# Expert stage of a fused scan, router and two feed-forward kernel: the order of routing work, written-out TensorE rounds, and split turns of the half tiles

## The reference

```python
for t in range(S):                      # 4 batches, 8 heads, 768 tokens, head size 48
    cur = einsum('bhd,bhe->bhde', u[None] * kt, vt)
    y[:, :, t] = einsum('bhd,bhde->bhe', rt, state + cur)
    state = wt[:, :, :, None] * state + einsum('bhd,bhe->bhde', kt, vt)
...
noisy = x @ w_gate + log1p(exp(x @ w_noise)) * noise   # x: 3072 x 384, 8 experts
top2, top2_w = the two best experts of each token, softmax over the two
for e in range(8):
    out[mask] += top2_w * (maximum(x[mask] @ w1[e], 0) @ w2[e])   # 384 -> 1024 -> 384
...
h = x @ w_in                            # 384 -> 2048
return (h - tanh(h)) @ w_out            # 2048 -> 384
```

## Time and profile before

| | us |
|---|---|
| median of 3 runs | 1153.69 (1153.0 to 1162.76) |
| the profiled execution, its own time | 1157.02 |
| its span | 1155.4 |
| TensorE busy | 1076.8 (93% of the span), 8738 matmuls |
| VectorE, ScalarE, GpSimd busy | 702.6, 542.3, 199.2 |

### The profile page before, as it was taken

One profiled execution on the slowest core, in us unless ns is written; L12 is line 12 of the kernel. 1 busy time (PEld: TensorE's weight loads), 2 busy tenths in 40 slices (PEclk: granted clock), 3 DMA queues, 4 the chain that ended last, 5 costly groups with the idle time before them and its releaser, 6 DMA issues.

```text
span 1155.4 us, 24252 instructions
## 1 busy us (share of the span) xinstructions
PE 1076.8 (93%) x8738; PEld 1029.8 (89%) x8738; DVE 702.6 (61%) x892; ACT 542.3 (47%) x754; POOL 199.2 (17%) x325
## 2 busy tenths in 40 slices
PE   4887968998999999999999999899999999999998
PEld 3776866997999999999999999799999999999997
DVE  8978876489677777776776777543434344333433
ACT  4344424564466666666666666333332332323232
POOL 2108675017800000000000000401010110101010
PEclk9989889999899999999999999999999999999999
DMA  7645535859888888888888888301010110101010
GB/s 128 157 101 125 138 102 179 271 161 328 271 282 281 272 286 272 283 274 271 275 273 273 274 276 285 99 14 62 1 61 0 61 55 6 61 0 61 0 61 20
DMA packets 121067, 184.99 MB, mean 160 GB/s; under 512 B 12176, under 2 KB 84112, under 8 KB 121008
## 3 DMA queue, kind: packets, MB, share of 16 engines
q1 hardware_dynamic: 106016, 152.44, 43.3%
q0 software_dynamic: 6528, 20.06, 5.2%
q10 hardware_dynamic: 8464, 11.70, 2.9%
HBM read 156.85 MB, written 27.33 MB: 159 GB/s over the span
## 4 chain that ended last, share of the span: by engine, by line
PE 79%; DVE 9%; POOL 5%; issue 4%; ACT 2%; DMA 1%; ACTq 0%; DVEq 0%; POOLq 0%; SPq 0%
PE ps L761 6%; PE ps L850 6%; PE ps L849 6%; PE ps L830 6%; PE ps L832 6%; PE ps L831 6%; PE ps L848 6%; PE ps L763 6%; PE ps L762 6%; PE ps L719 5%; PE ps L721 5%; PE ps L720 5%; PE ps L739 2%; PE ps L738 2%; PE ps L737 2%
## 5 line engine op out<-in xcount | busy, mean ns | idle before, releaser
L1470 DVE TENSOR_TENSOR w_lo<-w_raw,w_hi 128x1536 fp32r<-128x1536 f32 x140 | 244.2, 1754 | 87.8 <-ACT w_hi L886 87.6
L886 ACT ACTIVATE w_hi<-w_raw 128x1536 fp32r<-128x1536 f32 x140 | 206.6, 1488 | 18.5 <-ACT y_out L1048 12.0
L1878 POOL DMA_INDIRECT yy<-yg,slot_g x54 | 54.2, 1004 | 733.9 <-DVE w_lo L1470 408.1
L1470 DVE TENSOR_TENSOR gg<-ps,th 128x768 f32<-128x768 f32 x64 | 61.3, 957 | 167.8 <-ACT th L1095 167.8
L761 PE MATMUL ps<-w_hi,h_hi 128*128 128x384 f32 x440 | 150.0, 341 | 9.0 <-DVE h_lo L1540 8.3
L719 PE MATMUL ps<-xT_hi,w_hi 128*128 128x256 f32 x480 | 139.7, 291 | 11.1 <-DVE xT_lo L1470 5.8
L763 PE MATMUL ps<-w_hi,h_lo 128*128 128x384 f32 x440 | 147.1, 334 | 0.0
L762 PE MATMUL ps<-w_lo,h_hi 128*128 128x384 f32 x440 | 147.0, 334 | 0.0
L721 PE MATMUL ps<-xT_hi,w_lo 128*128 128x256 f32 x480 | 137.3, 286 | 0.0
L720 PE MATMUL ps<-xT_lo,w_hi 128*128 128x256 f32 x480 | 137.2, 286 | 0.0
L848 PE MATMUL ps<-wout_hi,g_hi 128*128 128x384 f32 x384 | 130.4, 340 | 0.0
(11 more groups left out here) (286 smaller groups left out, 2027.8 us busy)
## 6 DMA issues: line engine op xcount, KB each, us to landing
w_raw<-in_moe_w SPq DMA_DIRECT2D x140, 768.0 KB, 5.4
xt_in<-xg SPq DMA_DIRECT2D x20, 384.0 KB, 4.3
yg<-y_out ACTq DMA_DIRECT2D x20, 384.0 KB, 6.0
klin<-in_k_cols SPq DMA_DIRECT2D x32, 144.0 KB, 3.8
v_nat<-in_v_pairs SPq DMA_DIRECT2D x16, 288.0 KB, 3.5
out<-o_out SPq DMA_DIRECT2D x8, 576.0 KB, 4.0
wz<-in_w_cols SPq DMA_DIRECT2D x30, 144.0 KB, 3.7
rlin<-in_r_cols SPq DMA_DIRECT2D x28, 144.0 KB, 3.7
```

What stands on the lines that cost most here:

```text
L886: nc.scalar.activation(dst, src, ACT.Copy).then_inc(s, 1)
L1470: vec.tensor_tensor(dst, a, b, ALU.subtract).then_inc(s, 1)
```

## The change

Five parts.

- **PE, DVE and ACT, whole tiles.** The pieces of routing and tables move to other places. The first transpose of batch 3's rows stands ahead of `up(whole(0))`, its second logits end `down(whole(0))`; the places 5 and 6 of PE are now in the middle and at the end of `down`. `ranks` moves from tile 2, block 0, to the middle of tile 1's `down`; `spell(0)` from block 1 of tile 3 to ahead of its `down`; `spell(1)` from block 0 of tile 4 to block 1 of the first round. On DVE there are places 0 (start of a tile) and 7 (its end), the router's pieces come one or two places earlier, and the tables are spread from tile 2 to the first round.
- **DVE.** `describe` is cut in two, `rows_told` and `rest_told`, so that `singles_2` becomes `singles_2` and `singles_3`. The instructions are the same.
- **SP.** The weights of whole(4) and of two_parts(0) are issued ahead of the wait for the scatters, w2's second half of whole(4) ahead of table_ready 3. The rows of one_part(0) are loaded after table_ready 4 as before.
- **PE, rounds.** All 15 rounds are written out; no hardware loop, waits are on constants.
- **Half tiles.** `turn_h(i, 0)` moves into `up_rows`, ahead of the last three matmuls of half 1, and ACT does h_row and h_hi of half 0 before h_row and h_hi of half 1.

```diff
@@ -487,12 +487,22 @@
             clear_pads()
+            sp.wait_ge(w2_lo_s, 2 * whole(3).n + 2)
+            load_w2(whole(4), 1)
             sp.wait_ge(table_ready, 3)
+            for hf in range(2):
+                sp.wait_ge(w1_lo_s, 2 * whole(3).n + 3 + hf)
+                load_w1(two_parts(0), hf)
+            sp.wait_ge(w2_lo_s, 2 * whole(3).n + 3)
+            load_w2(two_parts(0), 0)
             sp.wait_ge(padded, 16 * (E + 1))
             sp.wait_ge(scattered[1], 16 * JB * 2 * 2)
-            tile_loads(whole(3), whole(4), two_parts(0), None)
+            sp.wait_ge(xT_full, whole(3).n + 2)
+            load_x(two_parts(0))
+            sp.wait_ge(w2_lo_s, 2 * whole(4).n + 2)
+            load_w2(two_parts(0), 1)
             sp.wait_ge(table_ready, 4)
-            tile_loads(whole(4), two_parts(0), one_part(0), None)
+            tile_loads(whole(4), None, one_part(0), None)
             for t in (two_parts(NSING - 1), one_part(NSING - 1)):
...
@@ -737,6 +747,8 @@
                         mm = pe.matmul(o, xT_hi[:, c, 0:TS], w1_lo[:, c, cols], start=False, stop=(c == KD - 1))
+                        if hf == 1 and c == KD - 2:
+                            turn_h(s, 0)
                     mm.then_inc(h_full, FC // 4)
...
@@ -745,7 +757,7 @@
 
-            def down(t):
+            def down(t, step=lambda place_: None):
                 pe.wait_ge(y_copied, t.n)
...
@@ -763,15 +775,14 @@
                         mm.then_inc(y_half, 1)
+                        step(FC // 2 + 1)
                 mm.then_inc(y_full, 1)
+                step(FC // 2 + 2)
 
             last = B - 1
-            between = {(0, 0): [lambda: rows_in_turn(last, 0, 0)], (0, 1): [lambda: rows_in_turn(last, 0, 1)],
-                       (0, 2): [lambda: rows_in_turn(last, 0, 2)], (0, 3): [lambda: rows_in_turn(last, 1, 0)],
-                       (0, 4): [lambda: logits(last, 0), lambda: rows_in_turn(last, 1, 1)],
-                       (1, 0): [lambda: rows_in_turn(last, 1, 2)], (1, 1): [lambda: logits(last, 1)],
-                       (2, 0): [lambda: ranks(2, lg_taken, B)],
-                       (3, 1): [lambda: spell(0)], (4, 0): [lambda: spell(1)]}
+            between = {(0, 0): [turns(last, 0, 1)], (0, 1): [turns(last, 0, 2)], (0, 2): [turns(last, 1, 0)],
+                       (0, 3): [lambda: logits(last, 0), turns(last, 1, 1)], (0, 5): [turns(last, 1, 2)], (0, 6): [lambda: logits(last, 1)],
+                       (1, 5): [lambda: ranks(2, lg_taken, B)], (3, 4): [lambda: spell(0)], (5, 1): [lambda: spell(1)]}
 
...
@@ -786,27 +797,21 @@
             turn_tile(whole(0))
+            rows_in_turn(last, 0, 0)
             for k_ in range(NA):
-                up(whole(k_), lambda b, k_=k_: first_step(k_, b))
+                up(whole(k_), lambda at, k_=k_: first_step(k_, at))
                 turn_tile(whole(k_ + 1) if k_ + 1 < NA else two_parts(0))
                 first_step(k_, FC // 2)
-                down(whole(k_))
-            with pe.Fori(0, NSING - 1) as i:
-                up(two_parts(i))
+                down(whole(k_), lambda at, k_=k_: first_step(k_, at))
+            for i in range(NSING):
+                up(two_parts(i), lambda at, i=i: first_step(NA + i, at))
                 turn_tile(one_part(i))
...
                 up_rows(one_part(i), i)
-                turn_h(i, 0)
-                turn_tile(two_parts(i + 1), after_one=i)
+                if i + 1 < NSING:
+                    turn_tile(two_parts(i + 1), after_one=i)
                 turn_h(i, 1)
                 down(one_part(i))
-            up(two_parts(NSING - 1))
-            turn_tile(one_part(NSING - 1))
-            down(two_parts(NSING - 1))
-            up_rows(one_part(NSING - 1), NSING - 1)
-            turn_h(NSING - 1, 0)
-            turn_h(NSING - 1, 1)
-            down(one_part(NSING - 1))
 
...
@@ -1002,7 +1007,6 @@
                     nc.scalar.activation(h_row[:, hf, :], ps[:, 2 + hf, :], ACT.Relu).then_inc(h_rows, 1)
-                for hf in range(2):
                     reg_wait(act, h_turned, 2 * s + 1 + hf)
...
@@ -1049,9 +1053,9 @@
 
-            between = {(0, n + 1): [lambda n=n: keep_rows(B - 1, n // KD, n % KD, X)] for n in range(4)}
-            between |= {(0, 6): [lambda: keep_rows(B - 1, 1, 1, X)], (1, 1): [lambda: keep_rows(B - 1, 1, 2, X)],
-                        (1, 3): [lambda: smooth(2, 0)], (1, 4): [lambda: smooth(2, 1)], (1, 5): [lambda: smooth(2, 2)],
+            between = {(0, n): [lambda n=n: keep_rows(B - 1, n // KD, n % KD, X)] for n in range(1, 5)}
+            between |= {(0, 6): [lambda: keep_rows(B - 1, 1, 2, X)],
+                        (1, 0): [lambda: smooth(2, 0)], (1, 1): [lambda: smooth(2, 1)], (1, 3): [lambda: smooth(2, 2)],
                         (2, 0): [lambda: smooth(2, 3)]}
...
@@ -1059,11 +1063,13 @@
             xT_high(whole(0))
+            keep_rows(B - 1, 0, 0, X)
             w2_high(whole(0), 0)
...
                 tile_act(whole(k_), whole(k_ + 1) if k_ + 1 < NA else two_parts(0), None, lambda at, k_=k_: first_step(k_, at))
+            act.wait_ge(table_ready, 3)
+            tile_act(two_parts(0), one_part(0), 0)
             act.wait_ge(table_ready, 4)
-            tile_act(two_parts(0), one_part(0), 0)
             tile_act(one_part(0), two_parts(1), 1)
...
@@ -1300,7 +1306,7 @@
 
-            def describe(rows, size, fills):
+            def rows_told(rows, size, fills):
 
...
@@ -1310,6 +1316,9 @@
                 seq(vec.tensor_reduce(enough[:, int(fills):int(fills) + 1], flat(4, rows), AX.X, ALU.max))
+
+            def rest_told(rows, size, fills):
+
                 seq(vec.tensor_tensor(r3(1, rows), r3(1, rows), b8(shift_r, rows), ALU.add))
...
@@ -1357,7 +1367,10 @@
             def singles_2():
-                describe(DS, TS, True)
+                rows_told(DS, TS, True)
+
+            def singles_3():
+                rest_told(DS, TS, True)
                 vec.memset(tick[:, 6:7], 0.0).then_inc(spelled, 1)
...
@@ -1532,6 +1545,7 @@
             def tile_dve(t, nxt, st, step=lambda k_: None):
+                step(0)
                 if t.one:
...
@@ -1562,12 +1576,13 @@
                     w2_low(nxt, 0)
-
-            between = {(1, 2): [lambda: take(B - 1), lambda: softplus_1(2)], (1, 3): [lambda: softplus_2(2)],
-                       (1, 4): [lambda: softplus_3(2)], (1, 5): [lambda: choose_1(2)], (1, 6): [lambda: choose_2(2)],
-                       (2, 1): [lambda: placed(2), lambda: slots(2), counts], (2, 2): [lambda: weights(2)], (2, 3): [late[0]], (2, 4): [late[1]], (2, 6): [late[2]],
-                       (3, 2): [lambda: entered(0)], (3, 3): [late[3]], (3, 4): [late[4]], (4, 1): [lambda: entered(1)],
-                       (4, 2): [tiles_enough]}
+                step(7)
+
+            between = {(1, 0): [lambda: take(B - 1), lambda: softplus_1(2)], (1, 1): [lambda: softplus_2(2)], (1, 2): [lambda: softplus_3(2)],
+                       (1, 3): [lambda: choose_1(2)], (1, 4): [lambda: choose_2(2)], (1, 6): [lambda: placed(2), lambda: slots(2), counts],
+                       (2, 1): [parts_1], (2, 3): [lambda: weights(2)], (2, 6): [pairs_1], (2, 7): [pairs_2],
+                       (3, 4): [lambda: entered(0)], (3, 6): [singles_1], (4, 2): [singles_2], (4, 6): [singles_3],
+                       (5, 2): [lambda: entered(1)], (5, 6): [tiles_enough]}
 
...
@@ -1577,7 +1592,7 @@
                 tile_dve(whole(k_), whole(k_ + 1) if k_ + 1 < NA else two_parts(0), None, lambda at, k_=k_: first_step(k_, at))
-            tile_dve(two_parts(0), one_part(0), 0)
+            tile_dve(two_parts(0), one_part(0), 0, lambda at: first_step(NA, at))
             tile_dve(one_part(0), two_parts(1), 1)
...
```

More of the change, by code:

```diff
@@ L1349, in pairs_2 @@
             def pairs_2():
-                describe(DP, T, False)
+                rows_told(DP, T, False)
+                rest_told(DP, T, False)
                 vec.memset(tick[:, 6:7], 0.0).then_inc(spelled, 1)
@@ L1377, in tiles_enough @@
                 vec.tensor_copy(enough_i[:], enough[0:1, 2:3]).then_inc(enough_s, 1)
-            return early_1, early_2, counts, (parts_1, pairs_1, pairs_2, singles_1, singles_2), entered, tiles_enough
+            return early_1, early_2, counts, parts_1, pairs_1, pairs_2, singles_1, singles_2, singles_3, entered, tiles_enough
         @block.vector
@@ L1466, in states @@
                                        0.0, ALU.add, ALU.mult).then_inc(S_ready, 1)
-            early_1, early_2, counts, late, entered, tiles_enough = tables(v_)
+            early_1, early_2, counts, parts_1, pairs_1, pairs_2, singles_1, singles_2, singles_3, entered, tiles_enough = tables(v_)
             def sub(dst, a, b, s):
```

## The result

The changed kernel is slower: 1171.92 us median of 4 runs (1168.07 to 1177.72) against 1154.26 of 4 runs of the kernel before on the same chip, ratio 1.014, 95% interval 1.009 to 1.020. The forecast was 1150.6, with 1159 as its upper end. The profiled execution took 1171.72 (span 1170.2), 14.8 us of span more than the one before.

The account below looks back on a forecast made before the run. PE, busy 93% of the span, was taken as the bound, by its work and idle time. Whole tiles and first round gain 9.2 us, rounds lose 6.1: 3.1 faster, 1150.6 us at the median's level, range 1140 to 1159.

Parts of the forecast that it names:

- Part 1: Whole tiles: PE's four idle times behind DVE go, 8.7 us, plus 2.0 of half clock and 0.3, less 0.5 stall.
- the last issue falls near 281 instead of 287.23: Scatters ahead of load_x(two_parts(0)): they begin some 6 us earlier, so their last issue was to come earlier too.
- No stall, up to 1.5 if it slips: Rows of two_parts(0), before their turns: there near 290, wanted by PE near 291; at most 1.5 us of waiting.
- Part 2: First round: table_ready 4 now comes there, so PE stalls 1.3 us before turn_tile(one_part(0)), bounds 0 to 2.5.
- land at 13 to 16 and are wanted at 19: hidden: First round's half-tile weights, issued behind its rows: there in time, no cost; times in us from `up`.
- Part 3: Rounds without the hardware loop: taken alone, 0.37 us gained for each of 13 edges, 4.8 us.
- Part 4: Split turns in half tiles: next `up` 0.78 us later, 0.41 with the loop edge gone; 6.1 us lost in all.
- a first `up` after 305: Sign in the changed profile: the first round's `up`, forecast near 300 instead of 311.5, coming after 305 would refute Part 1.
- A: Rival, half tiles: h_row in time, both stalls gone (11.3 us), plus 4.8 from the loop and 9.2: 1128.4 us; 6%.
- B: Rival, rounds: the split is neutral and the loop's edges go, 14.0 us gained: 1139.7 us; 13%.
- D: Rival, written-out rounds: code loading, 20 more instruction packets each stopping PE for a us: 1170.6 us; 4%.
- C: Rival: the first part gives only some 4 us as the two load_x come later; rounds lose 6: 1155.7 us; 13%.

Follow-up runs that it names:

- e12: e10 with the low parts of the weights of tiles 1 to 5 made zeros by a one-input operation; 1187.21 us, ratio 1.013 to the kernel before.
- e11: e10 with load_x(two_parts(0)) ahead of that tile's first three weight loads; 1175.18 us, ratio 1.003 to the kernel before.
- e14: The kernel of e11 run once more, on a chip that has the stretch as well; 1179.21 us, kernel before 1179.61 there.
- e4: Changed kernel with the split turns undone, new order and written-out rounds kept; 1176.84 us, ratio 1.000 to the kernel before.
- e6: Changed kernel with the pieces of the last layer's weights started one tile later; 1186.51 us, ratio 1.008 to the kernel before.
- e10: Changed kernel with the last tables made earlier and `spell(1)` in the middle of tile 4's `down`; 1163.25 us, ratio 1.005 to the kernel before.
- e1: Kernel before with its 15 rounds written out and nothing else; 1168.32 us, ratio 0.994 to the kernel before.
- e2: Kernel before with the split turns alone, the loop kept; 1184.8 us, ratio 1.010 to the kernel before.
- e9: Changed kernel, split undone, staged pieces one tile later, turn_tile(two_parts(0)) in mid-`down`, tables as in e10, zero stores behind half-tile loads; 1143.78 us, ratio 0.990 to kernel before.
- the third group: The unaltered changed kernel, e10 and e9 on a chip of the result's kind; ratios 1.012, 1.005 and 0.990 to the kernel before (1155.15 us).
- e15: The kernel of e12 run once more on another chip; 1193.3 us, kernel before 1179.61 there.

## Why the prediction was wrong

The forecast was 3.1 us faster; the span was 14.8 longer. The 17.9 between them, by the prediction's own steps. (One trace is compared with one: the second trace of the changed kernel has `up(whole(0))` at 200.7 instead of 203.7 and 105.6 us of whole tiles instead of 106.8, so terms of a microsecond there are within what two executions differ by.)

- **Part 1, the idle times of DVE: right.** Without the new wait the whole tiles would have gained 1.5 + 9.4 = 10.9 us; the forecast for that stretch was 8.7 + 2.0 - 0.5 and 0.75 for the spell that leaves it, 10.9.
- **Part 1, "the last issue falls near 281 instead of 287.23": wrong, and the step that turned the sum.** The scatters start 5.1 earlier, as forecast, but I took their 33.4 us for a constant of POOL. It was 23 times 1.27, 3.6 us of waiting for DVE and 0.6 of small delays, and the change adds 5.5 of waiting to that. Of these 3.3 are the gain itself: tile 4's own w_lo, which in the kernel before ran from 287.85 on, when the last scatter had begun, now come 10 to 13 us earlier, at 275.18, 277.79 and 281.90, and hold the scatters of 276.32, 278.07 and 282.02 (1.45, 2.30 and 2.48 us). e12 shows the mechanism.
- **"No stall, up to 1.5 if it slips": wrong by 7.7 and 1.7 of half clock.** Of the 9 us between the rows' forecast 290 and 299, 6 are the later last issue; the rest is the landing: SP issues its next load 8.8 behind the last scatter's issue, at 296.17, where in the kernel before it did so 4.3 behind, at 291.48. That this is owed to the weights beside it is argued, not shown (e11 and e14 stayed open). The last packets of the scatters' queue end 7.6 us behind the last issue here and 3.1 in the kernel before, but only 2.4 and 2.3 in e4 and e6, whose loads stand in the same order, on chips with the stretch.
- **Part 2, "land at 13 to 16 and are wanted at 19: hidden": wrong by 4.9.** The weights did come at 12.4 and 15.8. What was left out is the rest of SP's and ACT's program order behind table_ready 4: three stores of zeros, then the staged piece, which landed at 20.5 and which ACT must take before y_out. The stall of 1.3 that I did forecast did not come; one of 4.67 came a step later, and half the clock went with it (1.65). e6 and e10 show both parts of that.
- **Part 3: right.** 0.35 for an edge, forecast 0.37 (e1). The Trainium skill's 51 ns for a plain branch (Advanced Engine Details and Errata, Control Flow Timing), weighed in the prediction, is not what an edge costs here.
- **Part 4: the mechanism right in every step, a size off.** The split was to cost 0.78 a round and cost 0.92; with the edge's gain 0.41 was to be left and 0.56 was. With round 0 that is 1.7 us.
- The start and the end took 1.9 more than forecast: 0.8 ahead of `up(whole(0))` and 1.1 behind the rounds. At the start PE's idle time ahead of `up` fell from 1.85 to 1.21, as the transpose fills it, but `up` waits for ACT's xT_hi, 2.73 us behind the turns of its rows as before, the rows come 0.5 later, and the clock stayed at half (0.50 over 203.60 to 207.84). No run asked for the rest.

9.4 + 4.9 + 1.7 + 1.9 = 17.9. By its own sign, a first `up` after 305, part 1 was wrong (310.5). Of the rivals, A and B fell on the split (e2), D on e1. C named the right place in part: load_x(two_parts(0)) came later than counted, while in round 0 the rows were in time and the weights and the staged piece were late. It priced this as 5 us of missing gain, where it was 9.4 and 4.9; its chance of 13% was too small for a step whose only cover was "near 290" against "near 291".

## What to carry to other kernels

When tiles run earlier against a series of GpSimd DMA issues, the two meet anew. Such a series has no fixed length: count VectorE's long SBUF operations that will be running when an issue starts. And where a load becomes late, read the consumer's whole queue in program order (a small staged piece held y_out, h_row and PE), and put what depends on a late count last in it, or in the middle of a long `down`, as in e9.

## What the runs showed of the hardware

- A scatter issue (0.96 us) beside a two-input VectorE subtraction of 1.75 us took up to 2.48, and each that started while one ran ended 0.83 to 0.85 behind its end (9 in the changed kernel, 5 in the one before); one that started first took 0.96 to 1.07. Without the subtraction 24 of them took 30.3 us instead of 38.7. A one-input operation of 0.95 us held one in the same way (1.59).
- A loop edge on PE costs its 0.35 us also where the first instruction behind it waits for data later than that: the two add (29.35 against 28.43 with a loop, 28.99 against 28.07 without).
- 13 rounds more of written-out code cost nothing: 56 instruction packets instead of 37, and rounds 0.35 us shorter.
- Behind idle times of 7.56 and 4.67 us TensorE's granted clock was 0.53 and 0.50, behind those of 0.35 to 0.73 in the rounds 1.00.
- On four of the chips all engines but GpSimd nearly stand while its scatters are issued back to back, 10 us in most kernels and about 20 in the two whose scatters were held least (tile 2 36.6 and 39.2 us). Not so on the chips of the result and of the third group, and the cause is open. These two, e12 and e15, were slower than e11 and e14 beside them.
